# One more split step in a fused attention and two-MLP kernel, with the high parts of three split steps made by VectorE

## The reference

```python
qn = q / (np.linalg.norm(q, axis=1, keepdims=True) + 1e-06)
kn = k / (np.linalg.norm(k, axis=1, keepdims=True) + 1e-06)
s = kn.transpose(0, 2, 1) @ qn / tau          # 256 x 256
a = softmax over the last axis of s
x = v @ a                                     # 6016 x 256
h = x @ moe_w_in;  x = (h * sigmoid(1.702 * h)) @ moe_w_out
h = x @ moe2_w_in; out = elu(h) @ moe2_w_out
```

## Time and profile before

| what | value |
|---|---|
| median of three runs | 1028.24 us |
| the profiled execution's own time | 1028.24 us |
| span of its instructions | 1026.5 us |
| TensorE busy | 1021.6 us |
| VectorE busy | 762.3 us |
| ScalarE busy | 760.4 us |
| GpSimd busy | 37.0 us |
| TensorE clock granted | 1.00 in all of it |

### The profile page before, as it was taken

The page is one execution under the profiler, slowest core; times in us unless marked ns, Lnnn a source line. Parts: engine busy times, 40 slices in busy tenths (PEclk is TensorE's granted clock), DMA queues, the critical chain, the costliest instruction groups (busy, mean ns, idle before and its releaser), DMA issues.

```text
span 1026.5 us, 14103 instructions
## 1 busy us (share of the span) xinstructions
PE 1021.6 (100%) x4650; PEld 861.5 (84%) x4650; DVE 762.3 (74%) x1247; ACT 760.4 (74%) x1364; POOL 37.0 (4%) x39
## 2 busy tenths in 40 slices
PE   9999999999999999999999999999999999999998
PEld 8988888888888888889998888888888888888997
DVE  6897756565656565655888988887888788788776
ACT  7996665575666566556688888888888788888875
POOL 6800000000000000000000000000000000000000
PEclk9999999999999999999999999999999999999999
DMA  9921012002003002003113002102102000110111
GB/s 360 306 41 42 1 42 42 1 36 47 1 1 80 1 1 60 1 1 124 42 62 99 1 1 62 21 1 62 21 1 62 9 14 24 35 21 1 21 22 36
DMA packets 103434, 46.25 MB, mean 45 GB/s; under 512 B 87170, under 2 KB 94018, under 8 KB 102722
## 3 DMA queue, kind: packets, MB, share of 16 engines
q1 hardware_dynamic: 100816, 44.38, 15.7%
q10 hardware_dynamic: 2546, 0.98, 0.4%
HBM read 33.03 MB, written 12.32 MB: 44 GB/s over the span
## 4 chain that ended last, share of the span: by engine, by line
PE 98%; DMA 1%; POOL 0%; SPq 0%; DVE 0%; issue 0%; ACT 0%; DVEq 0%
PE bank L1241 32%; PE bank L1242 32%; PE bank L1243 32%; PE bank L1251 1%; DMA qk<-in_k_dram 1%; POOL qk_lo L472 0%; PE bank L1356 0%; PE bank L1357 0%; PE bank L1361 0%; SPq L362 0%; PE bank L1334 0%; PE bank L1501 0%; PE bank L1264 0%; DVE blocks L1220 0%; DVE xo L1230 0%
## 5 line engine op out<-in xcount | busy, mean ns | idle before, releaser
L1241 PE MATMUL bank<-g_hi,w_dn_hi 128*128 128x512 f32 (+1 forms) x768 | 296.2, 386 | 0.1
L1242 PE MATMUL bank<-g_lo,w_dn_hi 128*128 128x512 f32 (+1 forms) x768 | 295.8, 385 | 0.0
L1243 PE MATMUL bank<-g_hi,w_dn_lo 128*128 128x512 f32 (+1 forms) x768 | 295.7, 385 | 0.0
L992 DVE TENSOR_TENSOR g_lo<-gated,g_hi 128x512 fp32r<-128x512 f32 (+1 forms) x384 | 259.4, 677 | 47.6 <-ACT g_hi L667 41.7
L1241 PE MATMUL bank<-blk_hi,w_up_hi 128*128 128x512 f32 (+1 forms) x672 | 259.0, 385 | 0.0
L1243 PE MATMUL bank<-blk_hi,w_up_lo 128*128 128x512 f32 (+1 forms) x672 | 258.9, 385 | 0.0
L1242 PE MATMUL bank<-blk_lo,w_up_hi 128*128 128x512 f32 (+1 forms) x672 | 258.8, 385 | 0.0
L667 ACT CAST g_hi<-gated 128x512 fp32r<-128x512 f32 (+1 forms) x289 | 176.3, 610 | 20.5 <-DVE gated L979 20.4
L1241 PEld LDWEIGHTS bank<-g_hi,w_dn_hi 128*128 128x128 f32 x768 | 144.2, 188 | 28.3 <-DVE g_lo L992 1.1
L1243 PEld LDWEIGHTS bank<-g_hi,w_dn_lo 128*128 128x128 f32 x768 | 144.2, 188 | 27.0
L1242 PEld LDWEIGHTS bank<-g_lo,w_dn_hi 128*128 128x128 f32 x768 | 144.2, 188 | 26.6
(11 more groups left out here) (130 smaller groups left out, 777.5 us busy)
## 6 DMA issues: line engine op xcount, KB each, us to landing
x_scratch<-xo SPq DMA_DIRECT2D x10, 512.0 KB, 3.1
raw<-x_scratch SPq DMA_DIRECT2D x5, 1024.0 KB, 5.6
out_dram<-blocks SPq DMA_DIRECT2D x40, 128.0 KB, 2.8
qk<-in_q_dram SPq DMA_DIRECT2D x12, 384.0 KB, 10.4
qk<-in_k_dram SPq DMA_DIRECT2D x12, 384.0 KB, 11.1
stage<-in_moe_w_in_dram SPq DMA_DIRECT2D x8, 512.0 KB, 8.1
stage<-in_moe_w_out_dram SPq DMA_DIRECT2D x8, 512.0 KB, 3.9
blocks<-in_v_dram SPq DMA_DIRECT2D x32, 128.0 KB, 3.3
```

The lines of the kernel that those rows point to most:

```text
L992: nc.vector.tensor_tensor(g[1][:, x, 0:w], gated[:, n % 2, 0:w], g[0][:, x, 0:w].bitcast(F32), ALU.subtract).then_inc(c_glo, 1)
L1241: nc.tensor.matmul(out_ps, w_hi, x_hi, start=start, stop=False, skip_group_check=goes_on)
L1242: nc.tensor.matmul(out_ps, w_hi, x_lo, start=False, stop=False, skip_group_check=goes_on)
L1243: return nc.tensor.matmul(out_ps, w_lo, x_hi, start=False, stop=stop, skip_group_check=goes_on)
```

## The change

`TWICE` gets group 13, so step (13,1) is done in three split matmuls for each half instead of whole. That adds a high part and a low part to be made. The new list `CAST_BY_VECTOR` names groups 6, 10 and 13: the high parts of (6,1), (10,1) and (13,1) are now made by VectorE, in its loop over the sums, just ahead of the sum of the same group. POOL waits for them by a new semaphore `c_qkhi3`. It still makes the high parts of (4,1), (8,1), (12,1) and (14,1).

```diff
-    TWICE = [4, 6, 8, 10, 12, 14]
+    TWICE = [4, 6, 8, 10, 12, 13, 14]
+
+    CAST_BY_VECTOR = [6, 10, 13]
...
             for i, (n, step) in enumerate(SPLITS):
-                if step:
+                if step and n in CAST_BY_VECTOR:
+                    pool.wait_ge(c_qkhi3, CAST_BY_VECTOR.index(n) + 1)
+                elif step:
                     pool.wait_ge(c_qk[n % RING], qk_count(n))
                     if i >= PARTS:
                         pool.wait_ge(c_score, SPLITS[i - PARTS][0] + 1)
                     nc.gpsimd.tensor_copy(qk_hi[:, i % PARTS, :, :], qk[:, n % RING, :, step, :]).then_inc(c_qkhi2, 1)
-                    pool.wait_ge(c_qkhi2, TWICE.index(n) + 1)
+                    pool.wait_ge(c_qkhi2, [m for m in TWICE if m not in CAST_BY_VECTOR].index(n) + 1)
...
             for n in range(LANES):
+                if n in CAST_BY_VECTOR:
+                    i = SPLITS.index((n, 1))
+                    dve.wait_ge(c_qk[n % RING], qk_count(n))
+                    if i >= PARTS:
+                        dve.wait_ge(c_score, SPLITS[i - PARTS][0] + 1)
+                    nc.vector.tensor_copy(qk_hi[:, i % PARTS, :, :], qk[:, n % RING, :, 1, :]).then_inc(c_qkhi3, 1)
                 dve.wait_ge(c_sq, n + 1)
```

More of the change, by code:

```diff
@@ L177, in attention_and_two_mlps @@
         c_qkhi2 = sem("c_qkhi2")
+        c_qkhi3 = sem("c_qkhi3")
         c_qklo = sem("c_qklo")
```

## The result

The changed kernel took 1030.86 us (median of nine runs, 1029.96 to 1032.76), against 1028.24 us before (1027.89 to 1029.48): a ratio of 1.0026, with an interval of 1.0016 to 1.0037. That is 2.6 us more. Run once more beside other kernels it gave 1030.78 us against 1028.49, a ratio of 1.0020 (1.0011 to 1.0029). The forecast was 1029.5 us with a range up to 1030.8; the measured time lies just above that range. It is also on the far side of the 0.2% line (1030.3), though the interval reaches down to 1.0016 and the second measurement stands on the line itself. These ratios and intervals, and those further down, are as they were measured over all runs, and can differ a little from the quotient of two medians.

A forecast was written before the change was run, and what follows sets the result against it. The prediction took POOL's low parts to bound the kernel up to 17.12 us and TensorE afterwards. A delay of 1.38 less a gain of 0.14 gave 1028.24 + 1.24, or 1029.5 us, range 1028.7 to 1030.8.

The forecast's parts named there:

- What bounds the kernel: Start of the first stage: POOL's low parts, with its cast of (6,1), bound until 17.12 us, TensorE after that.
- part 2: VectorE's cast of (6,1) comes behind its sum of group 5, so TensorE starts (6,0) 1.38 us late, not recovered.
- Part 1: Extra split step in group 13: TensorE takes 2.30 us instead of 2.44, a gain of 0.14 us.
- Part 3: POOL after (6,1): two casts fewer, one low part more; last low part ends at 41.66, hidden by 0.45 us.
- The cover of 0.45 us: Margin by which POOL's last low part (18,0) would still be ready before TensorE wants it at 42.16.
- Rival 1: VectorE's casts and POOL's subtractions cannot overlap: 0.54 us late at groups 10 and 13 each, 1030.1 us, chance 0.25.
- Part 4: VectorE's later sums, the squares, high parts and folds behind them, and POOL's weight low parts: all costed at nothing.
- Parts 4 and 5: Part 4, and loads from group 15 on, issued up to 1.38 us later but landing well before use: no cost.
- Rivals 2 and 3: Rival 2; and the other, that the delay is hidden and only the 0.14 us gain stays: 1028.1 us, chance 0.08.
- Rival 2: TensorE's clock falls to half in the new gap before (6,0), costing 1.5 us more: 1031.0 us, chance 0.08.

The follow-up runs named there:

- e3: Kernel before with only VectorE's cast of (6,1), behind its sum of group 5, and no further split step: 1030.34 us against 1028.44, ratio 1.0017.
- e5: Changed kernel with VectorE's cast of (6,1) ahead of its sum of group 5 instead of behind it: 1029.27 us against 1028.49, ratio 1.0006.
- e2: Changed kernel with VectorE's first weight subtraction waiting until POOL has made all its low parts: 1029.88 us against 1028.44, ratio 1.0012.
- e4: Kernel before with two unread VectorE instructions, a copy ahead of the sum of group 8 and a subtraction ahead of that of group 12: 1029.38 us, run once.
- e1: Kernel before with only the further split step at group 13, POOL making all high parts of step 1: 1029.31 us against 1028.44, ratio 1.0015.
- after_again: The changed kernel, unaltered, run once more beside other kernels: 1030.78 us against 1028.49, ratio 1.0020.
- after: The changed kernel in its first measurement, against the kernel before: 1030.86 us against 1028.24, ratio 1.0026.
- e6: e5 with the wait of e2, and ScalarE's high part of (6,0) ahead of its square of group 6: 1029.22 us against 1028.49, ratio 1.0008.

## Why the prediction was wrong

**What bounds the kernel, and part 2 (the cast of (6,1)): right.** Forecast 1.38 us for (6,0); 1.36 in the changed kernel, 1.37 at the norms of e3. It reached the norms in full, and one place earlier in VectorE's order it vanishes (e5). The cast took the 0.42 us of the row that I had taken.

**Part 1 (the gain of 0.14 us): right** on TensorE's row, group 13 at 2.30 us.

**Part 3 (POOL afterwards): this step failed.** It said that the last low part ends at 41.66, hidden by 0.45 us. It ended at 43.14, or 43.28 by the clock of before, 1.6 us later. The sum had POOL and VectorE work side by side without touching. In the changed kernel (10,1) starts at 24.32 against my 24.05, which with the earlier start of 0.14 is 0.41 us of lateness; the four low parts around (13,1) add 0.17 more (28.73 to the cast of (14,1) at 33.88, 5.15 us, against 28.47 to 33.43, 4.96, and 0.02 of rounding; it is the low part of (12,0) that is long); the last one adds 1.03. Take the last away (e2) and TensorE's loss falls from 2.50 to 1.50 us, close to the 1.24 that the forecast had. The cover of 0.45 us was the term that failed with it: 1.6 us of lateness less 0.45 is 1.2 us on top of the 1.24 forecast.

**Rival 1 had the mechanism, but two of its three places.** I gave it 0.25 and the time 1030.1. It put 0.54 us on each of two casts, measured 0.41 and 0.17, and missed the third meeting, VectorE's weight subtraction at the end. Part 4 names that subtraction, ended at 41.50, and costs it at nothing since POOL's own weight work comes later; it doesn't compare it with POOL's last `qk_lo`, which part 3 puts at 40.4 to 41.66, into the same time. Before, the two missed each other by 0.4 us: POOL ended at 39.92, VectorE began at 40.28. Part 4 also left VectorE's start at 40.28, and it was 40.78. The meeting alone measured 1.0 us. With all three meetings as measured the forecast's own sum gives 1028.24 + 1.24 + 1.63 - 0.45 = 1030.66, 0.2 us under the measured time.

The Trainium skill, page "SBUF — State Buffer", section "Who interferes with whom", gives this rule with both kinds of instruction: a copy in a two-port mode, and an instruction with two SBUF inputs against a GpSimd instruction that reads SBUF. The probe agrees with each: 0.96 us for a copy (none ran alone; the cast of that shape takes 0.42), and 2.14 and 2.26 us for a subtraction and a low part that take about 1.2 and 1.29 alone. I had weighed only its first half.

**Parts 4 and 5 (squares, folds, loads): right** as far as the traces show; no wait of TensorE in the profile of the changed kernel is for them. But the way over VectorE's late sums to POOL, which part 4 costs at nothing, is a real one: the probe e4 pushed it to 0.62 us. **Rivals 2 and 3:** in the profiled executions the clock stayed at 1.00 around the new waits, and nothing was hidden. Rival 2 is not settled for the few slowest runs, with their mean clock of 0.998.

**The size of the change in time.** Of the 2.50 us at the norms in the first profile, 1.00 goes with the last meeting (e2), and the late cast less the gain on group 13 makes 1.24 of the other 1.50. The 0.26 left shows in e2's timeline of TensorE. The last low part is still late: the row before it starts at 42.34 and the one that reads it at 42.61, 0.27 us for a step that runs in 0.12 otherwise, and the rows from there to the norms take 0.81 us instead of 0.72. Group 14, with 2.35 us, has 0.05 more. The other outcome of the meeting leaves 1.58 in all.

## What to carry to other kernels

A step handed from a busy engine to another one starts when that engine's order gets to it, not when its input is there: read the instruction ahead of it in the new order first. One place in the order moved the waiting matmul by 1.4 us here, and the cast itself takes 0.4. And when an engine gets later by an instruction, list what else begins in the time it now reaches into; a pair of instructions that just missed each other before (by 0.4 us here) can meet. The view of the chain that ended last doesn't show such a meeting as a wait; compare the lengths of like instructions instead.

## What the runs showed of the hardware

VectorE and POOL took turns at instruction length, in either order. VectorE's subtraction of 1.22 us took 1.36 to 2.40 us behind a low part of POOL, by how early it came, and ended 1.07 or 1.08 us after POOL's in all five profiles in which it was second (e1, e3, e4, e5, after_again). A copy or cast of 128x512 that had to wait ended 0.28 or 0.29 us after POOL's (after, after_again, e2, e4, e5, e6), and a low part of 1.29 us, which took 1.47 to 2.34 behind VectorE, ended 1.14 to 1.16 us after VectorE's (after, after_again, e2, e4). The time of waiting is inside the row of the instruction that waits. Which goes first changed between two executions of one program in which both began within 0.02 us, and moved its norms by about 0.9 us. VectorE's sums of three steps, with one input in PSUM, kept their 1.75 to 1.77 us throughout.
